# Where VectorE writes the outer product of a step, where ScalarE copies the minus half, and which load goes first: three moves in a fused DFT and two-layer MoE kernel

## The chip, the cores and the metric

The kernel runs on one core of one Trainium2 chip. The metric is the device time of one execution in microseconds (us). Shorter is better. The engines are TensorE (PE), VectorE (DVE), ScalarE (ACT), GpSimd (POOL) and the queue engine SyncE (SP), which issues nearly all DMAs.

## What is computed

```python
X = np.fft.fft(x, axis=1)            # x: 2 x 3008 x 256, fp32
X = np.fft.fft(X, axis=2).real
h = X.reshape(6016, 256) @ w_in1     # 256 -> 2048
y = relu(h)**2 @ w_out1              # 2048 -> 256
h = y @ w_in2
P = a0 + a1*h + a2*h*h + a3*h*h*h
Q = 1 + |b0|*|h| + |b1|*h*h
out = (P / (Q + 1e-6)) @ w_out2
```

## The kernel before, in words

**The transform.** The real part of the 2D DFT is symmetric, so only 3012 columns are worked on: the transform gives two sums per column, and a column and its mirror are `plus + minus` and `plus - minus` in the first layer's hidden values. A matmul in full fp32 is not used: each operand is split into a high part and a low rest (`hi`, `lo`), and each product is three matmuls (lo\*hi, hi\*lo, hi\*hi).

**Tiles and steps.** The columns are 12 tiles of 256 (the last has 196). A tile with its mirror gives 512 tokens. The 2048 hidden values are 16 blocks of 128, taken two at a time, so a tile has 8 units and the kernel has 96 steps (`STEPS`). Step s makes the first layer's unit s, and, ten steps later (`SKEW`), the second layer's unit of the same number. All engines run the same step number side by side from orders that are written out by hand; nothing is scheduled by a planner.

**TensorE in step s** (in this order): `up1(s)`, 12 matmuls of 256 columns, first the minus half (L884), then the plus half (L892); `down1(s-2)`, 12 matmuls of 512 (L868); `up2(s-10)`, 12 matmuls of 512 (L859); `down2(s-12)`, 12 matmuls of 512 (L868). The plus half accumulates onto an outer product that VectorE has written into the same PSUM bank, so it waits for `outer_ready`. `up2` waits until VectorE has read the previous unit's result (`h2_read`), since the second layer's hidden values have one pair of PSUM banks.

**VectorE in step s**: add and subtract of plus and minus (L718, L719), which give the hidden values of 512 tokens; `divide(s-11)`, three instructions (L736, L738: two steps to the reciprocal, L742: the quotient); `outer_product(s+1)`, two instructions (L690); every eighth step `keep_z_lo` (L747), the low part of the first layer's output; `read_h2(s-10)`, three instructions (L725 makes q', L726 and L728 the cubic; L728 is the last reader of the PSUM banks). In steps 0 to 10 `divide` has nothing to do; there the outer product stands directly behind the subtract, and `split1` (L757) makes the low part of the hidden values.

**ScalarE in step s**: ReLU and square (L549, L551), every eighth step `keep_z_hi` (L606), `abs_h2` and `cubic_h2` (L567, L575), which read `up2`'s result, `keep_hi1` (L558), every eighth step `keep_out` (L613), then |q'| (L581), the copy of the next step's minus half out of PSUM (`keep_minus`, L543), and logarithm and exponential (L591, L594), the seed of the reciprocal.

**GpSimd in step s**: the split of the quotient into high and low (L498, L500) as soon as VectorE's L742 is done, then the low part of the first layer's hidden values (L491). Before step 10 it splits the second layer's weights, which come by two DMAs of 2 MB: eight pairs of L463 and L465. TensorE waits for the first four pairs ahead of step 10 and for all eight ahead of step 12.

**SyncE** stores the transform's tiles, and once the last is stored it loads tile 1 back (`load_y(1)`, two DMAs), then the second layer's two weights. The later tiles are loaded from the step loop.

The order of the middle of a step, on VectorE and on ScalarE:

```python
                if before is not None:
                    divide(before)
                if before is not None and unit(s + 1) is not None:
                    outer_product(s + 1)
```

```python
                if second is not None:
                    abs_q(second)
                if unit(s + 1) is not None:
                    keep_minus(s + 1)
                ...
                if second is not None:
                    seed_from_q(second)
```

Of the kernel before, what the change touches and what calls it, by code (L numbers as in the profile page):

```python
# [62 lines left out]
EARLY = TILES - 2  # L63
# [68 lines left out]
def fft_moe_kernel(nc, x, w_in1, w_out1, w_in2, w_out2, coef, f47, fold, twiddle, pair, out_t):  # L132
# [9 lines left out]
    with ctx:  # L142
# [105 lines left out]
        def unit(m):  # L248

            return m if 0 <= m < STEPS else None  # L250

        def pairs(t):

            return min(WIDE, COLUMNS - t * WIDE)
# [67 lines left out]
        def y_of(t):  # L322

            return y_odd if t % Y_BUFS else y_even
# [40 lines left out]
        def after_u_stored(eng, t):  # L365
            eng.wait_ge(u_stored[t % (STAGE_BUFS + 1)], 16 * (t // (STAGE_BUFS + 1) + 1))
# [4 lines left out]
        def _(sp):  # L371
# [3 lines left out]
            def load_w(dst, w, loaded):  # L375
                sp.dma_start(dst[:, :, :], w.rearrange("(k p) f -> p k f", p=P)).then_inc(loaded, 16)
# [13 lines left out]
            def load_y(t):  # L390
                n = pairs(t)
                for v, s in zip(y_d, y_of(t)):
                    sp.dma_start(s[:, :, 0:n].bitcast(F32), v[:, :, t * WIDE:t * WIDE + n]
                                 ).then_inc(y_loaded[t % Y_BUFS], 16)
# [6 lines left out]
            def load_u(t):  # L401
                n = pairs(t)
                after_u_stored(sp, t)
                sp.dma_start(u_s[:, t % Y_BUFS, 0:n], u_d[:, t * WIDE:t * WIDE + n].to_broadcast([P, n])
                             ).then_inc(u_loaded[t % Y_BUFS], 16)

            def store_out(t):
                n = 2 * pairs(t)
                sp.wait_ge(out_kept, t + 1)
                if t < TILES - 1:  # L410
                    sp.dma_start(out_v[:, :, t * TN:t * TN + n], out_s[:, :, 0:n]).then_inc(out_stored, 16)
                    return
                sp.dma_start(out_v[:, 0, t * TN:t * TN + n], out_s[:, 0, 0:n]).then_inc(out_stored, 16)
                sp.wait_ge(upper_kept, 1)
                sp.dma_start(out_v[:, 1, t * TN:t * TN + n], out_s[:, 1, 0:n]).then_inc(out_stored, 16)
# [18 lines left out]
                after_stored(sp, t)  # L434
            for t in range(TILES - STAGE_BUFS - 1, TILES):
                after_u_stored(sp, t)
            load_y(1)
            load_w(w_in2_raw, w_in2, w_in2_loaded)
            load_w(w_out2_raw, w_out2, w_out2_loaded)
            for t in range(1, TILES):  # L440
                sp.wait_ge(plus_ready, t * UNITS)
                if t + 1 < TILES:
                    load_u(t + 1)
                    load_y(t + 1)
                if t >= 3:
                    store_out(t - 3)
# [67 lines left out]
        def _(act):  # L514
# [25 lines left out]
            def keep_minus(m):  # L540
                act.wait_ge(minus_ready, m + 1)
                after(act, diff_done, m)
                nc.scalar.activation(minus_s[:, :, 0:pairs(m // UNITS)], h1_minus(m), ACT.Copy).then_inc(minus_kept, 1)  # L543
# [64 lines left out]
            def keep_out(t):  # L608
                n = 2 * pairs(t)
                after(act, out_stored, 16 * t)  # L610
                if t < TILES - 1:
                    act.wait_ge(prod2_done, (t + 1) * UNITS)
                    nc.scalar.activation(out_s[:, :, 0:n], o_p[:, :, 0:n], ACT.Copy).then_inc(out_kept, 1)  # L613
                else:
                    act.wait_ge(half_done, 1)
                    nc.scalar.activation(out_s[:, 0, 0:n], o_p[:, 0, 0:n], ACT.Copy).then_inc(out_kept, 1)
# [10 lines left out]
            for s in range(STEPS):  # L627
                second, summed, multiplied = unit(s - SKEW), unit(s - LAG1), unit(s - SKEW - LAG2)
                square_relu(s)
                if summed is not None and summed % UNITS == UNITS - 1:  # L630
                    keep_z_hi(summed // UNITS)
                if second is not None:
                    from_h2(second)
                if s >= HEAD:
                    keep_hi1(s)
                if multiplied is not None and multiplied % UNITS == UNITS - 1:
                    keep_out(multiplied // UNITS)
                if second is not None:
                    abs_q(second)
                if unit(s + 1) is not None:  # L640
                    keep_minus(s + 1)
                if s == 0:
                    keep_y_hi(EARLY)
                if second is not None:
                    seed_from_q(second)
                if s < HEAD:
                    keep_hi1(s)
                if s == 0:
                    keep_y_hi(EARLY + 1)
# [19 lines left out]
        def _(dve):  # L669
# [13 lines left out]
            def outer_product(m):  # L683
                t, n = m // UNITS, pairs(m // UNITS)
                if m % UNITS == 0:
                    dve.wait_ge(u_loaded[t % Y_BUFS], 16 * (t // Y_BUFS + 1))
                after(dve, diff_done, m)
                for i in range(2):
                    f = 2 * (m % UNITS) + i
                    nc.vector.tensor_scalar(h1_plus(m)[:, i, :], u_s[:, t % Y_BUFS, 0:n], w_col[:, f:f + 1], None, ALU.mult  # L690
                                            ).then_inc(outer_ready, 1)

            def keep_y_lo(t):
                hi, lo = y_tile(t)
                dve.wait_ge(y_hi_kept, t + 1)
                if t > STAGE_BUFS:
                    after_u_stored(dve, t - STAGE_BUFS - 1)
                nc.vector.tensor_copy(u_stage[:, t % (STAGE_BUFS + 1), 0:pairs(t)], uv_bank(t)[0:1, 1, :]).then_inc(u_kept, 1)
                nc.vector.tensor_tensor(lo, uv_bank(t), hi.bitcast(F32), ALU.subtract).then_inc(y_lo_kept, 1)
# [60 lines left out]
            for s in range(STEPS):  # L760
                second, before, summed = unit(s - SKEW), unit(s - SKEW - 1), unit(s - LAG1)
                add_and_subtract(s)
                if before is None:
                    outer_product(s + 1)
                if s == 1:
                    keep_y_lo(EARLY)
                if 0 < s <= HEAD:
                    split1(s - 1)
                if s == 1:
                    keep_y_lo(EARLY + 1)  # L770
                if before is not None:
                    divide(before)
                if before is not None and unit(s + 1) is not None:
                    outer_product(s + 1)
                if summed is not None and summed % UNITS == UNITS - 1:
                    keep_z_lo(summed // UNITS)
                if second is not None:
                    read_h2(second)
# [219 lines left out]
```

## Time and profile before

| | |
|---|---|
| median of 3 runs | 1044.0 us (1040.78 to 1044.02) |
| the profiled execution's own time | 1043.1 us |
| its span | 1041.3 us |
| TensorE busy, matmul / weight load | 1003.2 us (96%) / 848.1 us |
| VectorE busy | 941.8 us (90%) |
| ScalarE busy | 882.0 us (85%) |
| GpSimd busy | 572.1 us (55%) |
| chain that ended last, by engine | DVE 45%, ACT 28%, issue 15%, PE 9%, POOL 2%, DMA 1% |
| DMA engines, mean share | high in the first 95 us only |

A matmul's end in the profile is modelled and overlaps the next one's start (a 512-column matmul shows 0.39 us and the next starts some 0.23 us behind it), so TensorE's progress is read from the starts. The first step's add starts at 70 us; the steps up to 10 take 4.1 to 4.5 us each, those from 14 on 9.7 us, every eighth of them 10.8 us; behind 954 us the last units of the second layer are drained.

### The profile page before, as it was taken

The numbers are of one execution on the slowest core, as the hardware profiler recorded it, in microseconds if no ns is written. First come the engines' busy times: TensorE is split into PE (matmuls) and PEld (weight loads), VectorE is DVE, ScalarE is ACT, GpSimd is POOL, SyncE is SP. The second block draws the span as 40 slices with busy tenths as digits, with TensorE's granted clock in tenths as the row PEclk, the third lists the DMA queues.
The fourth block names the chain that finished last, engine by engine and source line by source line (L and its number), as shares of the span: only waits on it lengthen the run. The fifth ranks groups of instructions, "written<-read, shape, count | busy, mean of one in ns | idle before, by whom it ended". The sixth has DMA issues, their size and how long they took to land.

```text
span 1041.3 us, 13708 instructions
## 1 busy us (share of the span) xinstructions
PE 1003.2 (96%) x5098; PEld 848.1 (81%) x5098; DVE 941.8 (90%) x1040; ACT 882.0 (85%) x929; POOL 572.1 (55%) x305
## 2 busy tenths in 40 slices
PE   9999889999999999999999999999999999999875
PEld 8798778888888888888888888888888888788775
DVE  2368899999999999999999999999999999999997
ACT  2348879999899999899899999999999999898873
POOL 0143955656556556556556566566565565565342
PEclk9999989999999999999999999999999999999997
DMA  9766000001001001001001001001001000000000
GB/s 247 289 194 236 7 1 27 1 1 47 1 1 46 1 1 46 1 1 46 2 1 46 1 1 46 1 1 46 1 1 40 1 1 21 1 21 1 1 21 15
DMA packets 24174, 38.02 MB, mean 37 GB/s; under 512 B 1694, under 2 KB 18986, under 8 KB 23466
## 3 DMA queue, kind: packets, MB, share of 16 engines
q1 hardware_dynamic: 24060, 37.14, 11.3%
q8 instruction: 40, 0.66, 0.3%
q14 instruction: 26, 0.21, 0.1%
q10 hardware_dynamic: 48, 0.02, 0.0%
HBM read 25.31 MB, written 11.84 MB: 36 GB/s over the span
## 4 chain that ended last, share of the span: by engine, by line
DVE 45%; ACT 28%; issue 15%; PE 9%; POOL 2%; DMA 1%; DVEq 0%; ACTq 0%; SPq 0%
DVE den_s L725 9%; DVE den_s L738 9%; DVE den_s L736 9%; ACT seed_s L594 9%; ACT seed_s L591 8%; DVE g_value L742 8%; ACT minus_s L543 5%; DVE ps L690 4%; PE ps L805 3%; PE ps L825 2%; PE ps L814 1%; ACT g_value L575 1%; PE ps L868 1%; ACT g_value L549 1%; POOL w_in_lo L465 1%
## 5 line engine op out<-in xcount | busy, mean ns | idle before, releaser
L868 PE MATMUL ps<-g_hi,w_out_lo 128*128 128x512 f32 (+1 forms) x764 | 301.6, 395 | 17.3 <-POOL w_in_lo L500 8.0
L868 PE MATMUL ps<-g_hi,w_out_hi 128*128 128x512 f32 (+1 forms) x764 | 300.3, 393 | 0.0
L868 PE MATMUL ps<-g_lo,w_out_hi 128*128 128x512 f32 (+1 forms) x728 | 283.9, 390 | 0.0
L498 POOL CAST g_hi<-g_value 128x1024 fp32r<-128x1024 f32 x86 | 89.6, 1042 | 339.5 <-DVE g_value L742 339.5
L500 POOL TENSOR_TENSOR g_lo<-g_value,g_hi 128x1024 fp32r<-128x1024 f32 x86 | 207.3, 2411 | 6.9
L491 POOL TENSOR_TENSOR g_lo<-g_value,g_hi 128x1024 fp32r<-128x1024 f32 (+1 forms) x86 | 204.6, 2380 | 0.0
L868 PEld LDWEIGHTS ps<-g_hi,w_out_lo 128*128 128x128 f32 x764 | 145.9, 191 | 47.3 <-POOL w_in_lo L500 9.3
L868 PEld LDWEIGHTS ps<-g_hi,w_out_hi 128*128 128x128 f32 x764 | 145.2, 190 | 29.2
L868 PEld LDWEIGHTS ps<-g_lo,w_out_hi 128*128 128x128 f32 x728 | 137.9, 189 | 25.6
L581 ACT ACTIVATE den_s<-den_s 128x1024 f32<-128x1024 f32 x88 | 93.5, 1062 | 62.9 <-DVE den_s L725 62.8
L736 DVE SCALAR_TENSOR_TENSOR den_s<-den_s,seed_s 128x1024 f32<-128x1024 f32 x87 | 107.7, 1238 | 25.3 <-ACT seed_s L594 25.3
L859 PE MATMUL ps<-z_hi,w_in_lo 128*128 128x512 f32 x352 | 110.7, 395 | 8.4 <-DVE g_value L728 8.4
L725 DVE SCALAR_TENSOR_TENSOR den_s<-den_s,b_abs,ps 128x1024 f32<-128x1024 f32 x88 | 112.1, 1273 | 5.3 <-ACT g_value L575 5.0
L742 DVE SCALAR_TENSOR_TENSOR g_value<-g_value,coef_s,den_s 128x1024 f32<-128x1024 f32 x86 | 110.5, 1285 | 3.0
L728 DVE SCALAR_TENSOR_TENSOR g_value<-g_value,coef_s,ps 128x1024 f32<-128x1024 f32 x86 | 110.2, 1281 | 3.0
L738 DVE SCALAR_TENSOR_TENSOR den_s<-den_s,seed_s 128x1024 f32<-128x1024 f32 x87 | 108.6, 1249 | 3.0
L859 PE MATMUL ps<-z_lo,w_in_hi 128*128 128x512 f32 x352 | 109.0, 391 | 0.0
L859 PE MATMUL ps<-z_hi,w_in_hi 128*128 128x512 f32 x352 | 108.6, 390 | 0.0
L549 ACT ACTIVATE g_value<-g_value 128x1024 f32<-128x1024 f32 (+1 forms) x96 | 100.3, 1044 | 7.9 <-DVE g_value L719 7.5
L726 DVE TENSOR_TENSOR g_value<-g_value,ps 128x1024 f32<-128x1024 f32 x86 | 104.5, 1215 | 0.0
L567 ACT ACTIVATE den_s<-ps,coef_s 128x1024 f32<-128x1024 f32 x88 | 97.1, 1103 | 7.8 <-PE ps L859 7.8
L575 ACT ACTIVATE g_value<-ps,coef_s 128x1024 f32<-128x1024 f32 x86 | 103.1, 1199 | 0.0
(118 smaller groups left out, 1894.2 us busy)
## 6 DMA issues: line engine op xcount, KB each, us to landing
x_s<-x SPq DMA_DIRECT2D x16, 384.0 KB, 7.2
out_t<-out_s SPq DMA_DIRECT2D x11, 512.0 KB, 5.7
w_out_unsplit_lo<-w_out SPq DMA_DIRECT2D x2, 2048.0 KB, 18.4
tw_s<-twiddle SPq DMA_DIRECT2D x1, 3012.0 KB, 17.3
y_hi_dram<-y_stage_hi SPq DMA_DIRECT2D x10, 256.0 KB, 3.7
y_lo_dram<-y_stage_lo SPq DMA_DIRECT2D x10, 256.0 KB, 4.5
w_in_raw<-w_in SPq DMA_DIRECT2D x1, 2048.0 KB, 10.5
w_in_unsplit_lo<-w_in SPq DMA_DIRECT2D x1, 2048.0 KB, 9.9
```

The lines of the kernel that those rows point to most:

```text
L491: nc.gpsimd.tensor_tensor(g1_lo_s[:, p, :, 0:n], r_s[:, p, :, 0:n], g1_hi_s[:, m % 2, :, 0:n].bitcast(F32), ALU.subtract).then_inc(pool_lo ...
L500: nc.gpsimd.tensor_tensor(lo, g, hi.bitcast(F32), ALU.subtract).then_inc(g2_lo, 1)
L549: nc.scalar.activation(r, r, ACT.Relu).then_inc(relu_done, 1)
L575: nc.scalar.activation(num_of(m), h2_banks(m)[:, :, 0:width(m)], ACT.Identity, bias=a2, scale=a3).then_inc(cubic_done, 1)
L725: nc.vector.scalar_tensor_tensor(den, den, b_abs[:, 0:1], h2, ALU.add, ALU.mult).then_inc(q_signed, 1)
L726: nc.vector.tensor_tensor(num, num, h2, ALU.mult).then_inc(t_h_done, 1)
L728: nc.vector.scalar_tensor_tensor(num, num, a1, h2, ALU.add, ALU.mult).then_inc(h2_read, 1)
L736: nc.vector.scalar_tensor_tensor(den, den, Q_CONST, seed, ALU.add, ALU.mult).then_inc(t_done, 1)
L738: nc.vector.scalar_tensor_tensor(den, den, 2.0, seed, ALU.subtract, ALU.mult, reverse0=True).then_inc(rec_done, 1)
L742: nc.vector.scalar_tensor_tensor(num, num, a0, den, ALU.add, ALU.mult).then_inc(g2_done, 1)
L859: last = nc.tensor.matmul(h[:, i, 0:n], lhs, rhs, start=(j == 0), stop=(j == len(products) - 1))
L868: last = nc.tensor.matmul(acc[:, mb, 0:n], w[a][:, f, mb * P:(mb + 1) * P], g[c][:, i, 0:n], start=(f == 0 and j == 0), stop=(f == FB - 1 ...
```

## The change

Three moves. On VectorE, `outer_product(s + 1)` stands directly behind the subtract in every step, ahead of `divide`; in step 1 one low part of the transform's (`keep_y_lo`) comes behind `split1` instead of ahead of it. On ScalarE, `keep_minus(s + 1)` comes ahead of `abs_q`. On SyncE, the second layer's weights are loaded ahead of tile 1. No instruction is added, taken away or made larger.

```diff
             for t in range(TILES - STAGE_BUFS - 1, TILES):
                 after_u_stored(sp, t)
-            load_y(1)
             load_w(w_in2_raw, w_in2, w_in2_loaded)
             load_w(w_out2_raw, w_out2, w_out2_loaded)
+            load_y(1)
...
                     keep_out(multiplied // UNITS)
+                if unit(s + 1) is not None:
+                    keep_minus(s + 1)
                 if second is not None:
                     abs_q(second)
-                if unit(s + 1) is not None:
-                    keep_minus(s + 1)
...
                 add_and_subtract(s)
-                if before is None:
+                if unit(s + 1) is not None:
                     outer_product(s + 1)
-                if s == 1:
-                    keep_y_lo(EARLY)
                 if 0 < s <= HEAD:
                     split1(s - 1)
                 if s == 1:
+                    keep_y_lo(EARLY)
                     keep_y_lo(EARLY + 1)
                 if before is not None:
                     divide(before)
-                if before is not None and unit(s + 1) is not None:
-                    outer_product(s + 1)
```

VectorE's instructions from the subtract of step 11 on, before (`g_value` holds first-layer values in L718 and L719 and the second layer's numerator elsewhere; `ps` is PSUM):

```order
L719 TENSOR_TENSOR g_value<-ps,minus_s 128x2x256
L736 SCALAR_TENSOR_TENSOR den_s<-den_s,seed_s 128x1024
L738 SCALAR_TENSOR_TENSOR den_s<-den_s,seed_s 128x1024
L742 SCALAR_TENSOR_TENSOR g_value<-g_value,coef_s,den_s 128x1024
L690 TENSOR_SCALAR ps<-u_s,w_col 128x256 x2
L725 SCALAR_TENSOR_TENSOR den_s<-den_s,b_abs,ps 128x1024
L726 TENSOR_TENSOR g_value<-g_value,ps 128x1024
L728 SCALAR_TENSOR_TENSOR g_value<-g_value,coef_s,ps 128x1024
L718 TENSOR_TENSOR g_value<-ps,minus_s 128x2x256
```

and now, at the same place:

```order
L719 TENSOR_TENSOR g_value<-ps,minus_s 128x2x256
L690 TENSOR_SCALAR ps<-u_s,w_col 128x256 x2
L736 SCALAR_TENSOR_TENSOR den_s<-den_s,seed_s 128x1024
L738 SCALAR_TENSOR_TENSOR den_s<-den_s,seed_s 128x1024
L742 SCALAR_TENSOR_TENSOR g_value<-g_value,coef_s,den_s 128x1024
L725 SCALAR_TENSOR_TENSOR den_s<-den_s,b_abs,ps 128x1024
L726 TENSOR_TENSOR g_value<-g_value,ps 128x1024
L728 SCALAR_TENSOR_TENSOR g_value<-g_value,coef_s,ps 128x1024
L718 TENSOR_TENSOR g_value<-ps,minus_s 128x2x256
```

The pair L690 moved from between the quotient (L742) and L725 to between the subtract (L719) and L736.

ScalarE's instructions of the same step, before:

```order
L558 ACTIVATE g_hi<-g_value 128x1024
L581 ACTIVATE den_s<-den_s 128x1024
L543 ACTIVATE minus_s<-ps 128x512
L591 ACTIVATE seed_s<-den_s,ln_bias 128x1024
L594 ACTIVATE seed_s<-seed_s,exp_bias 128x1024
```

and now:

```order
L558 ACTIVATE g_hi<-g_value 128x1024
L543 ACTIVATE minus_s<-ps 128x512
L581 ACTIVATE den_s<-den_s 128x1024
L591 ACTIVATE seed_s<-den_s,ln_bias 128x1024
L594 ACTIVATE seed_s<-seed_s,exp_bias 128x1024
```

L543 and L581 changed places; nothing else moved on ScalarE.

## Rows read from the trace of the kernel before

**Rows 1.** A plain and a z step: length, PE, PEld, DVE, ACT, POOL busy, PEclk.
```profile
571.08:580.77 9.69, 9.69 (x50) 8.17 (x49) 9.31 (x12) 8.85 (x10) 5.82 (x4) 1.00 0.00 0
580.77:591.59 10.82, 10.38 (x51) 8.34 (x49) 10.44 (x12) 9.75 (x11) 6.97 (x4) 1.00 0.00 0
```
**Rows 2.** Timeline of VectorE, plain step: start, duration, engine, line, operation, [idle before <-releaser].
```profile
571.08 0.69 DVE L718 TENSOR_TENSOR g_value<-ps,minus_s 128x512 f32<-128x512 f32 x1
571.68 0.68 DVE L719 TENSOR_TENSOR g_value<-ps,minus_s 128x512 f32<-128x512 f32 x1
572.63 1.23 DVE L736 SCALAR_TENSOR_TENSOR den_s<-den_s,seed_s 128x1024 f32<-128x1024 f32 x1 [0.27 <-ACT seed_s L594]
...
575.16 1.28 DVE L742 SCALAR_TENSOR_TENSOR g_value<-g_value,coef_s,den_s 128x1024 f32<-128x1024 f32 x1
576.36 0.87 DVE L690 TENSOR_SCALAR ps<-u_s,w_col 128x256 f32<-128x256 f32 x2
577.13 1.27 DVE L725 SCALAR_TENSOR_TENSOR den_s<-den_s,b_abs,ps 128x1024 f32<-128x1024 f32 x1
...
580.77 0.68 DVE L718 TENSOR_TENSOR g_value<-ps,minus_s 128x512 f32<-128x512 f32 x1
```
**Rows 3.** Who waited for whom: total us, times, longest.
```profile
DVE den_s L736 <- ACT seed_s L594: 25.3, 86, 1.1
```
**Rows 4.** Timeline of ScalarE in the same step.
```profile
578.44 1.06 ACT L581 ACTIVATE den_s<-den_s 128x1024 f32<-128x1024 f32 x1 [0.78 <-DVE den_s L725]
579.41 0.58 ACT L543 ACTIVATE minus_s<-ps 128x512 f32<-128x512 f32 x1
```
**Rows 5.** Timeline of TensorE: the first matmul of `up2` behind a z step.
```profile
513.10 0.71 PE L859 MATMUL ps<-z_hi,w_in_lo 128*128 128x512 f32 x2 [0.68 <-DVE g_value L728]
```
**Rows 6.** Timeline of GpSimd, plain step.
```profile
566.81 1.04 POOL L498 CAST g_hi<-g_value 128x1024 fp32r<-128x1024 f32 x1 [3.79 <-DVE g_value L742]
...
570.30 2.41 POOL L491 TENSOR_TENSOR g_lo<-g_value,g_hi 128x1024 fp32r<-128x1024 f32 x1
576.50 1.05 POOL L498 CAST g_hi<-g_value 128x1024 fp32r<-128x1024 f32 x1 [3.79 <-DVE g_value L742]
```
**Rows 7.** Timeline of VectorE, step 11.
```profile
126.41 1.97 DVE L736 SCALAR_TENSOR_TENSOR den_s<-den_s,seed_s 128x1024 f32<-128x1024 f32 x1 [0.27 <-ACT seed_s L594]
128.41 3.25 DVE L738 SCALAR_TENSOR_TENSOR den_s<-den_s,seed_s 128x1024 f32<-128x1024 f32 x1
```
**Rows 8.** Timeline of GpSimd: first and last of the 16 weight splits, first L491.
```profile
93.60 1.04 POOL L463 CAST w_in_hi<-w_in_unsplit_lo 128x1024 fp32r<-128x1024 f32 x1 [29.26 <-DMA w_in_unsplit_lo<-w_in]
...
124.91 2.38 POOL L465 TENSOR_TENSOR w_out_lo<-w_out_unsplit_lo,w_out_hi 128x1024 fp32r<-128x1024 f32 x1
127.25 3.32 POOL L491 TENSOR_TENSOR g_lo<-g_value,g_hi 128x1024 fp32r<-128x1024 f32 x1
```
**Rows 9.** Timeline of TensorE, `up1(12)`: first minus matmul, first plus matmul.
```profile
127.34 0.38 PE L884 MATMUL ps<-y_odd_hi,w_in_lo 128*128 128x256 f32 x1 [1.52 <-POOL w_out_lo L465]
...
133.82 0.58 PE L892 MATMUL ps<-y_odd_hi,w_in_lo 128*128 128x256 f32 x1 [5.50 <-DVE ps L690]
```
**Rows 10.** Busy time by engine just behind that wait (columns as in Rows 1).
```profile
134.00:140.00 6.00, 6.00 (x19) 5.00 (x20) 5.70 (x6) 4.96 (x6) 4.82 (x3) 0.57 0.00 0
```
**Rows 11.** Timeline of the SP queue: the issues that change places.
```profile
82.72 0.36 SPq L393 DMA_DIRECT2D y_odd_hi<-y_hi_dram  x1
...
83.65 0.46 SPq L376 DMA_DIRECT2D w_in_unsplit_lo<-w_in  x1
```
**Rows 12.** DMA issues between 82 and 104 us: KB each, us to landing.
```profile
w_out_unsplit_lo<-w_out SPq DMA_DIRECT2D x1, 2048.0 KB, 14.8
```
**Rows 13.** Timeline of TensorE: `up1(8)`, the first reader of tile 1.
```profile
102.90 0.28 PE L884 MATMUL ps<-y_odd_hi,w_in_lo 128*128 128x256 f32 x1
```
**Rows 14.** Length from step 14's L718 to step 90's, on to 95's; L718 busy.
```profile
158.43:906.22 747.79, 51.73 (x77) 1.00 0.05 15
906.22:953.51 47.29, 2.80 (x6) 1.00 0.03 12
```

## The prediction

> **What bounds the kernel now.** I read the granted clock first (full in both steps below), then the busy times by step, VectorE's timeline, the waits, and the other engines' timelines beside it.
>
> Most of the time is 66 plain steps of 9.69 us and 10 steps of 10.82 us in which the first layer's output is split too (z steps): 66 x 9.69 + 10 x 10.82 = 747.7, and the trace has 747.79 us from step 14's add to step 90's [rows 14]. In a plain step TensorE is busy 9.69 of 9.69 us; in a z step it is not, 10.38 of 10.82 [rows 1]. That missing time stands ahead of `up2`, which waits for VectorE's L728, the last reader of the PSUM banks [rows 5]. So TensorE sets the plain steps, and VectorE the z steps, by 10.82 - 9.69 = 1.13 us each.
>
> VectorE can't catch up in the seven steps between. It stands still for 0.27 us ahead of L736 in every step [rows 2], 86 times, 25.3 us in all, until ScalarE's exponential is done [rows 3]. That wait closes a ring: L725, |q'|, the copy of the minus half, logarithm, exponential, L736, L738, L742, L690, L725. Going round takes one step, 9.69, the same as TensorE's. Two engines are level here, and a third is close: see the port below.
>
> **ScalarE's move.** Ahead of |q'| ScalarE idles 0.78 us for L725, and the minus copy behind it takes 0.58 [rows 4]. Ahead of |q'| the copy fits into the idle time, so the exponential ends some 0.48 earlier (the start-to-start time of L543). Cost nothing, cover 0.78 us.
>
> **VectorE's move.** L690 takes 576.36 to 577.13, 0.78 us [rows 2]. Behind the subtract it fills the 0.27 us hole, and what it has more lies where the exponential no longer waits. I count from the end of L742 (575.16 + 1.28 = 576.44). L725 starts 0.08 before that end, as L690 does now; L725 to the next L718 takes 580.77 - 577.13 = 3.64; L718 and L719 take 571.08 to 572.36, 1.28; L690 0.78 with 0.03 of gap. L736 could start at -0.08 + 3.64 + 1.28 + 0.81 = 5.65. L736 to the end of L742 takes 572.63 to 576.44, 3.81 [rows 2]. VectorE alone would go round in 9.46 us. The exponential is no bound: L725 ends at 1.2, and from |q'| to L736 it is now 578.44 to 582.32 (L736 one step on), 3.88, less 0.48: 4.6, a whole us ahead of 5.65.
>
> **The port between VectorE and GpSimd is what is late next.** GpSimd begins its cast 0.06 behind L742's end (576.50), and its three instructions go from 566.81 to 572.71, 5.90 us [rows 6], so it is done at 5.96. Now L736 comes at 572.63, when it is just over. In the new order it comes at 5.65, on top of L491. What that costs, step 11 shows: there L736, which takes 1.23 elsewhere, took 1.97, and L738 3.25, beside GpSimd [rows 7, 8]. L736 started at 126.41; less its 1.23 it began to work at 127.15, 0.14 before L465's end at 127.29. L738 began to work at 128.41 + 3.25 - 1.23 = 130.43, 0.14 before L491's end at 130.57. So L736 and L738 (two SBUF inputs each) don't share with GpSimd; they wait until 0.14 before its instruction's end. Then L736 works from 5.96 - 0.14 = 5.82, and the round is 5.82 + 3.81 = 9.63 us. Of the 0.27 us hole, only 0.06 is gained in a plain step. Bounds: 9.46 (no block), 9.77 (block to the very end).
>
> The Trainium skill says of this (SBUF — State Buffer, "Who interferes with whom") that a VectorE instruction with two SBUF inputs and a GpSimd instruction that reads SBUF take a shared pair of ports as a lock, and the later one fully blocks until the first has finished. The blocking agrees with step 11. Its "until finished", taken at the instruction's shown end, would make 9.77 of 9.63; step 11 and the present plain step (L736 starts 0.08 before L491's end and takes its usual 1.23) speak for the 0.14.
>
> In a z step L747 puts 1.13 us more on VectorE, not on GpSimd, so the port is long free: 9.46 + 1.13 = 10.59 us.
>
> Steps 14 to 90: 66 x 9.63 + 10 x 10.59 = 741.5, less than 747.8 by **6.3 us**. TensorE could do 76 x 9.69 = 736.4; it no longer sets the pace, it waits some 0.5 us in every z step and never else. Steps 90 to 95 are narrower in the first layer and take 9.46 each [rows 14] with no block (GpSimd's L491 is shorter): 5 x 0.24 = **1.2 us**. Behind step 95 nothing changes.
>
> **The start.** Steps 10 to 13 hang on GpSimd's weight splits. GpSimd waits 29.26 us for the first weights and starts at 93.60; the last split ends at 127.29, and TensorE stands 1.52 us for it [rows 8, 9]. The weights would be issued 0.93 us earlier (82.72 for 83.65 [rows 11]) and go ahead of tile 1's 512 KB. Lower bound 0.9; upper 0.9 plus a quarter of the 9.9 us that `w_in`'s 2048 KB took from issue (83.65) to GpSimd's start, for those 512 KB, 3.4. I take 2.0: the tile's transfer partly ran in the time the weights needed to get going. The splits end at 125.3.
>
> In step 11 TensorE then stood 5.50 us for L690, since it lay behind the three divide instructions that the port held up [rows 9]; behind that wait the granted clock was 0.57 over six us [rows 10], between the full 2.4 GHz and half, 1.2 GHz. Now L690 comes right behind the subtract, at 126.2. L491 runs 125.3 to 127.7, L736 takes the port at 127.5, L742 ends at 131.3, step 12's add starts at 131.3 - 0.08 + 3.64 = 134.9, and step 14's two rounds of 9.63 later, at 154.1. It was 158.43 [rows 14]: **4.3 us** less. With no gain from the weights, L742 ends at 132.98 as now, and by the same working it is 2.6 us.
>
> Tile 1 now comes last. `w_out`, issued right behind `w_in` at 84.1, landed 14.8 later, at 99 [rows 11, 12], with all of these transfers ahead of it; the same bytes in another order end at about the same time, so tile 1 is there at 99 to 100. `up1(8)` reads it at 102.90 [rows 13], perhaps 0.9 us earlier with the swap in step 1 (`split1` first lets TensorE go on earlier). Cost nothing, cover 2 to 4 us. The swap itself ends in front of GpSimd's splits and is worth nothing.
>
> **Sum.** 4.3 + 6.3 + 1.2 = 11.8 us. Against the profiled execution, 1043.1: 1031.3. The median is 0.9 higher: **1032**.
>
> **The rivals.**
> *The port doesn't block so near the end*, or GpSimd gets through earlier: then TensorE sets nearly every step, 736.4 for 741.5, 5 us more gain, 1027. For: VectorE alone needs only 9.46. Against: both long instructions of step 11. Chance 0.12.
> *The start loses its gain to the clock.* TensorE has two idle stretches at about 133 and 142 us (1.5 and 2.9 us, for GpSimd's and VectorE's results) where it had one of 5.5. If the clock falls as it did, six us at 0.57 cost up to 4: 1036. Chance 0.13.
> *The block lasts to the end of L491*: 9.77 in plain steps, 66 x 0.14 = 9.2 less gain: 1041, no change that could be measured. It is the outcome by the page's rule. The rows above speak against it. Chance 0.18.
> *Slower: ScalarE waits for TensorE.* The minus copy now stands ahead of |q'|, and it needs the first half of `up1(s+1)`, which TensorE does last in its step. If that half comes late, |q'|, logarithm and exponential come late, and L736 waits for them again. It decides once the exponential comes later than 5.82, that is with the copy more than 1.1 us behind the end of L725. Were it 1.35 late, plain steps would take 9.88: 66 x 0.25 = 16 us, 1048. Against it: today L543 shows no wait, and TensorE has no idle time ahead of that half in plain steps. Chance 0.08.
>
> The forecast has 0.49.
>
> **How the numbers follow.** 0.3% (3.1 us, about what a measurement of this kernel can tell from no change) puts the border at 1040.9. Faster: the forecast, the first two rivals, and a quarter of the third, 0.79. Same: the rest of the third, 0.13. Slower: 0.08. The range takes in the forecast with its bounds, 1027 less 2, and the third rival up to the border: 1025 to 1041.
>
> **What would show it.** L736's duration: above 1.23, near 1.4, in plain steps with no wait on the exponential. L742's end to L742's end: 9.63 in plain steps, 10.59 in z steps. ScalarE's idle time for L725 gone or far below 0.78. TensorE's first `up2` matmul idle 0.3 to 0.6 in z steps. GpSimd's first split at about 91.6. L690 of step 11 at 126 and no wait of 5.5 us on it. Step 14's add at 154. A plain step that is still 9.69 with L736 undisturbed would mean that TensorE sets it and the port reading was wrong; a wait ahead of L543 would mean the slower rival.

## The result and the profile after

The changed kernel takes **1032.3 us** (median of 4 runs, 1031.93 to 1032.47) where the kernel before takes 1043.4 beside it (1040.78 to 1044.02): the ratio is 0.9898, with a 95% interval of 0.988 to 0.9916. The forecast was 1032, range 1025 to 1041. The profiled execution has a span of 1030.7 us for 1041.3. Three single executions in the runs below took far longer than the others of their kernel (2.0 ms for the kernel before, 1107.63 us with the loads' order alone, 5.6 ms with both halves on ScalarE); they are in the medians but not in the ratios.

The page of the changed kernel, busy time by engine:

```profile
PE 1001.2 (97%) x5098; PEld 847.3 (82%) x5098; DVE 954.1 (93%) x1040; ACT 901.1 (87%) x929; POOL 571.7 (55%) x305
```

VectorE shows 12 us more busy time than before, with the same instructions. Those are not work. Most of them are L736, 116.5 us in 87 instructions for 107.7, as the next rows show; L757 has 2.8 more in the first ten steps, and L738 2.0 less. The lines behind L690 keep their numbers below line 760; TensorE's are three lower than before (L856 is `up2`, L865 `down`, L881 and L889 the two halves of `up1`).

**The plain step**, VectorE's timeline, answering to [rows 2]:

```profile
564.74 0.68 DVE L718 TENSOR_TENSOR g_value<-ps,minus_s 128x512 f32<-128x512 f32 x1
565.34 0.68 DVE L719 TENSOR_TENSOR g_value<-ps,minus_s 128x512 f32<-128x512 f32 x1
566.05 0.88 DVE L690 TENSOR_SCALAR ps<-u_s,w_col 128x256 f32<-128x256 f32 x2
566.84 1.41 DVE L736 SCALAR_TENSOR_TENSOR den_s<-den_s,seed_s 128x1024 f32<-128x1024 f32 x1
568.28 1.22 DVE L738 SCALAR_TENSOR_TENSOR den_s<-den_s,seed_s 128x1024 f32<-128x1024 f32 x1
569.54 1.28 DVE L742 SCALAR_TENSOR_TENSOR g_value<-g_value,coef_s,den_s 128x1024 f32<-128x1024 f32 x1
570.74 1.28 DVE L725 SCALAR_TENSOR_TENSOR den_s<-den_s,b_abs,ps 128x1024 f32<-128x1024 f32 x1
...
574.38 0.68 DVE L718 TENSOR_TENSOR g_value<-ps,minus_s 128x512 f32<-128x512 f32 x1
```

and GpSimd's beside it, answering to [rows 6]:

```profile
564.74 2.42 POOL L491 TENSOR_TENSOR g_lo<-g_value,g_hi 128x1024 fp32r<-128x1024 f32 x1
570.89 1.04 POOL L498 CAST g_hi<-g_value 128x1024 fp32r<-128x1024 f32 x1 [3.73 <-DVE g_value L742]
```

There is no idle time ahead of L736 any more, and no wait for the exponential (of 86 such waits 2 are left, 1.4 us together, both behind step 95's add); instead L736 takes 1.41 us for 1.23. Its median is 1.35. It starts at 566.84 while L491 runs until 567.16. Less its own 1.22 it began to work at 567.03, 0.13 us before L491's end. Between steps 12 and 90 there are 59 L736 that are longer than 1.25 us, and by the same working all began 0.12 to 0.15 us before L491's end. The step is 574.38 - 564.74 = 9.64 us.

**The z step** from TensorE's side, the first matmul of `up2` in the two steps behind one, answering to [rows 5]:

```profile
194.56 0.70 PE L856 MATMUL ps<-z_hi,w_in_lo 128*128 128x512 f32 x2 [0.25 <-DVE g_value L728]
...
204.36 0.62 PE L856 MATMUL ps<-z_hi,w_in_lo 128*128 128x512 f32 x2
```

The wait is 0.25 us for 0.68. From `up2` to `up2`, that tile has six distances of 9.69 us, one of 10.11 and one of 9.80 (194.56 to 204.36), together 78.05 us for about 78.65.

**The start.** VectorE's step 11 [rows 7], GpSimd's splits and first L491 [rows 8], TensorE's `up1(12)` [rows 9]:

```profile
126.05 0.88 DVE L690 TENSOR_SCALAR ps<-u_s,w_col 128x256 f32<-128x256 f32 x2
126.83 1.22 DVE L736 SCALAR_TENSOR_TENSOR den_s<-den_s,seed_s 128x1024 f32<-128x1024 f32 x1
128.08 1.23 DVE L738 SCALAR_TENSOR_TENSOR den_s<-den_s,seed_s 128x1024 f32<-128x1024 f32 x1
```

```profile
90.41 1.04 POOL L463 CAST w_in_hi<-w_in_unsplit_lo 128x1024 fp32r<-128x1024 f32 x1 [26.59 <-DMA w_in_unsplit_lo<-w_in]
...
124.29 2.42 POOL L491 TENSOR_TENSOR g_lo<-g_value,g_hi 128x1024 fp32r<-128x1024 f32 x1
```

```profile
126.98 0.39 PE L889 MATMUL ps<-y_odd_hi,w_in_lo 128*128 128x256 f32 x1 [0.56 <-DVE ps L690]
...
143.94 0.74 PE L856 MATMUL ps<-z_hi,w_in_lo 128*128 128x512 f32 x2 [2.35 <-DVE g_value L728]
144.53 0.92 PE L856 MATMUL ps<-z_lo,w_in_hi 128*128 128x512 f32 x2
145.24 1.06 PE L856 MATMUL ps<-z_hi,w_in_hi 128*128 128x512 f32 x2
```

TensorE's wait of 5.50 us for L690 is 0.56. GpSimd starts 3.2 us earlier, so L491 is past before L736 comes, and neither L736 nor L738 is held up. Further on TensorE stands 2.35 us at 143.94, and then two matmuls take 0.59, 0.71 and 0.85 us, start to start, where they take 0.46 at full clock. The granted clock is 1.00 from 141 to 143.9, and 0.50, the half clock, from 145 to 148.

By stages, between the starts of VectorE's L718 in the profiled executions (us). "Vector", "scalar" and "weights" are the three moves alone, described below:

| stretch | before | after | vector | scalar | weights | vector + scalar |
|---|---|---|---|---|---|---|
| start to step 10 | 114.4 | 114.2 | 114.2 | 114.9 | 114.0 | 114.4 |
| steps 10 to 14 | 44.06 | 40.41 | 42.07 | 44.94 | 40.79 | 42.89 |
| steps 14 to 90 | 747.79 | 742.98 | 742.69 | 745.22 | 747.75 | 742.86 |
| steps 90 to 95 | 47.29 | 45.85 | 45.89 | 46.65 | 47.28 | 45.91 |
| step 95 to the end | 87.8 | 87.3 | 87.2 | 87.7 | 85.7 | 86.9 |

The first and last rows have the same work in the same order (but for the swap in step 1 and the order of the loads) in all six and still differ by up to 2 us, so single profiled executions are compared by the rows between. The row of steps 10 to 14 holds the clock as well: step 13 took 10.77 us in the changed kernel and 10.62 with vector + scalar, behind a fall of the clock, and 9.58 with vector alone, where the clock stayed full.

### The profile page after: what moved, and what is told of

Read it like the earlier page. It is cut to its first block, busy times and chain, and to the rows that moved or that the text cites. A ratio compares the mean times of both kernels' runs of the same rounds, so it can differ in the third digit from the quotient of the medians.

```text
span 1030.7 us, 13708 instructions
## 1 busy us (share of the span) xinstructions
PE 1001.2 (97%) x5098; PEld 847.3 (82%) x5098; DVE 954.1 (93%) x1040; ACT 901.1 (87%) x929; POOL 571.7 (55%) x305
## 4 chain that ended last, share of the span: by engine, by line
DVE 47%; PE 41%; issue 10%; ACT 2%; DVEq 0%; ACTq 0%
PE ps L865 20%; PE ps L856 10%; DVE den_s L736 7%; DVE den_s L725 7%; DVE den_s L738 6%; DVE g_value L726 6%; DVE g_value L742 6%; DVE g_value L718 4%; DVE g_value L719 3%; DVE ps L690 3%; PE ps L802 3%; PE ps L889 3%; PE ps L881 3%; PE ps L822 2%; PE ps L811 1%
## 5 line engine op out<-in xcount | busy, mean ns | idle before, releaser
L865 PE MATMUL ps<-g_hi,w_out_lo 128*128 128x512 f32 (+1 forms) x764 | 300.9, 394 | 16.9 <-POOL w_in_lo L500 9.5
L865 PE MATMUL ps<-g_hi,w_out_hi 128*128 128x512 f32 (+1 forms) x764 | 299.8, 392 | 0.0
L865 PE MATMUL ps<-g_lo,w_out_hi 128*128 128x512 f32 (+1 forms) x728 | 283.2, 389 | 0.0
L498 POOL CAST g_hi<-g_value 128x1024 fp32r<-128x1024 f32 x86 | 89.5, 1041 | 333.2 <-DVE g_value L742 333.2
L500 POOL TENSOR_TENSOR g_lo<-g_value,g_hi 128x1024 fp32r<-128x1024 f32 x86 | 207.9, 2418 | 6.9
L491 POOL TENSOR_TENSOR g_lo<-g_value,g_hi 128x1024 fp32r<-128x1024 f32 (+1 forms) x86 | 203.5, 2367 | 0.0
L865 PEld LDWEIGHTS ps<-g_hi,w_out_lo 128*128 128x128 f32 x764 | 145.5, 190 | 47.4 <-POOL w_in_lo L500 10.8
L865 PEld LDWEIGHTS ps<-g_hi,w_out_hi 128*128 128x128 f32 x764 | 145.0, 190 | 29.2
L865 PEld LDWEIGHTS ps<-g_lo,w_out_hi 128*128 128x128 f32 x728 | 137.4, 189 | 25.5
L725 DVE SCALAR_TENSOR_TENSOR den_s<-den_s,b_abs,ps 128x1024 f32<-128x1024 f32 x88 | 112.4, 1277 | 6.7 <-ACT g_value L575 4.9
L736 DVE SCALAR_TENSOR_TENSOR den_s<-den_s,seed_s 128x1024 f32<-128x1024 f32 x87 | 116.5, 1339 | 1.4 <-ACT seed_s L594 1.4
L856 PE MATMUL ps<-z_hi,w_in_lo 128*128 128x512 f32 x352 | 110.9, 396 | 6.6 <-DVE g_value L728 6.6
L549 ACT ACTIVATE g_value<-g_value 128x1024 f32<-128x1024 f32 (+1 forms) x96 | 100.1, 1043 | 16.6 <-DVE g_value L719 14.8
L742 DVE SCALAR_TENSOR_TENSOR g_value<-g_value,coef_s,den_s 128x1024 f32<-128x1024 f32 x86 | 110.5, 1285 | 3.0
L856 PE MATMUL ps<-z_lo,w_in_hi 128*128 128x512 f32 x352 | 109.5, 393 | 0.0
L738 DVE SCALAR_TENSOR_TENSOR den_s<-den_s,seed_s 128x1024 f32<-128x1024 f32 x87 | 106.6, 1225 | 3.0
L856 PE MATMUL ps<-z_hi,w_in_hi 128*128 128x512 f32 x352 | 109.1, 391 | 0.0
L575 ACT ACTIVATE g_value<-ps,coef_s 128x1024 f32<-128x1024 f32 x86 | 103.2, 1200 | 0.0
L551 ACT ACTIVATE g_value<-g_value 128x1024 f32<-128x1024 f32 (+1 forms) x96 | 100.4, 1046 | 3.0
## 6 DMA issues: line engine op xcount, KB each, us to landing
w_in_raw<-w_in SPq DMA_DIRECT2D x1, 2048.0 KB, 10.7
```

Of the source, the lines that this page charges most:

```text
L491: nc.gpsimd.tensor_tensor(g1_lo_s[:, p, :, 0:n], r_s[:, p, :, 0:n], g1_hi_s[:, m % 2, :, 0:n].bitcast(F32), ALU.subtract).then_inc(pool_lo ...
L500: nc.gpsimd.tensor_tensor(lo, g, hi.bitcast(F32), ALU.subtract).then_inc(g2_lo, 1)
L551: nc.scalar.activation(r, r, ACT.Square).then_inc(g1_done, 1)
L575: nc.scalar.activation(num_of(m), h2_banks(m)[:, :, 0:width(m)], ACT.Identity, bias=a2, scale=a3).then_inc(cubic_done, 1)
L725: nc.vector.scalar_tensor_tensor(den, den, b_abs[:, 0:1], h2, ALU.add, ALU.mult).then_inc(q_signed, 1)
L736: nc.vector.scalar_tensor_tensor(den, den, Q_CONST, seed, ALU.add, ALU.mult).then_inc(t_done, 1)
```

## The experiments

All times are medians beside the kernel before on the same chip; the ratio to it follows with its interval.

### The three moves apart

**VectorE's move alone:**

```diff
                 add_and_subtract(s)
-                if before is None:
+                if unit(s + 1) is not None:
                     outer_product(s + 1)
...
                     divide(before)
-                if before is not None and unit(s + 1) is not None:
-                    outer_product(s + 1)
```

(with the swap in step 1).

> Only VectorE's move. Theory A (the idle time ahead of L736 is gone as soon as L690 lies in it; the exponential, even with the minus copy still behind |q'|, is ready 5.1 us behind L742's end, ahead of the port's 5.8): the step loop is as with the whole change, plain steps 9.63 to 9.70 us and the step behind a z step 9.45, some 5 us less from step 14 to 90; the 5.5 us wait of step 11 is gone, but the weight splits end at 127.3 as before, so the start gives 2 to 3 us. Sum: 1035 to 1036. Theory B (the exponential still ends the wait, and ScalarE's move is what frees VectorE): L736 waits again, the steps stay at 9.69 and 10.8, and only the start's 2 to 3 us come: 1041.

Measured: 1033.9 us, 0.9925 (0.9908 to 0.9943). Theory A in its mechanism, and 1 us below its range (steps 90 to 95 give 1.4 us that its sum leaves out). Steps 14 to 90 take 742.7 us, as with the whole change. ScalarE's move adds nothing to it.

**ScalarE's move alone:**

```diff
-                if second is not None:
-                    abs_q(second)
                 if unit(s + 1) is not None:
                     keep_minus(s + 1)
+                if second is not None:
+                    abs_q(second)
```

> Only ScalarE's move. Theory A (the ring through the exponential is cut from this side as well; VectorE then comes 5.65 us behind L742's end to the same port): L736 stretches to about 1.4 us, z steps and the step behind them together 20.2 us instead of 20.5, 4 to 5 us less from step 14 to 90, nothing at the start, since L690 still stands behind the divide instructions in step 11: 1037 to 1039. Theory B (the hole has to be filled by L690 to be worth anything): no change, 1043.

Measured: 1038.8 us, 0.9966 (0.9952 to 0.9981). Theory A in its mechanism. The VectorE timeline of this kernel, in a plain step and with L690 at its old place:

```profile
288.12 0.68 DVE L719 TENSOR_TENSOR g_value<-ps,minus_s 128x512 f32<-128x512 f32 x1
288.86 1.35 DVE L736 SCALAR_TENSOR_TENSOR den_s<-den_s,seed_s 128x1024 f32<-128x1024 f32 x1
```

L736 comes right behind the subtract and is held up by the port here as well. The waits of this kernel still have the exponential, though, 24 times for 86:

```profile
DVE den_s L736 <- ACT seed_s L594: 10.2, 24, 1.1
```

One step in eight is 10.1 us long, that behind the step in which ScalarE also copies the output out of PSUM (`keep_out`): there L736 waits 0.68 us for the exponential. With L690 ahead of L736 that step takes 9.64, so the copy is covered; without, it costs 0.4 us a tile. So the gain from step 14 to 90 is 2.6 us, not 4.8. (The profiled execution, 1041.19 us, is the slowest of the twelve, which go from 1037.1 up.)

**The order of the loads alone:**

```diff
-            load_y(1)
             load_w(w_in2_raw, w_in2, w_in2_loaded)
             load_w(w_out2_raw, w_out2, w_out2_loaded)
+            load_y(1)
```

> Only the loads' order. GpSimd's splits start 2 to 3 us earlier and end near 124.5. L491 of step 10 is then past before L738 needs the port, so TensorE's wait for L690 in step 11 shrinks from 5.5 us by about 2.5. The step loop is unchanged. Theory A (the start is worth what GpSimd's end moves): 1040 to 1041. Theory B (the start hangs on VectorE's order, the weights alone only move a wait): 1042 to 1043.5.

Measured: 1038.2 us, 0.9961 (0.9947 to 0.9976). That is more than either theory gave. Steps 10 to 14 take 3.3 us less. TensorE still waits 4.76 us for L690 in step 11, where about 3 were expected, but the port is nearly free:

```profile
126.14 1.47 DVE L736 SCALAR_TENSOR_TENSOR den_s<-den_s,seed_s 128x1024 f32<-128x1024 f32 x1 [0.27 <-ACT seed_s L594]
127.64 1.23 DVE L738 SCALAR_TENSOR_TENSOR den_s<-den_s,seed_s 128x1024 f32<-128x1024 f32 x1
```

L736 and L738 take 1.47 and 1.23 us for the 1.97 and 3.25 of [rows 7]. The earlier splits let L491 end at 126.53, just behind L736's start at 126.14, and so out of the divide instructions. The clock has a part too: it is back at 1.00 by 135, where before the change it was 0.50 until 139, and step 12 takes 10.57 us for 11.43. The step loop is unchanged at 747.75 us.

**VectorE's and ScalarE's moves, without the loads:**

> Everything but the loads' order. The weights' share is what this lacks against the whole change (1032.3). Theory A (splits end at 127.3, L736 takes the port ahead of L491 and L738 is held up behind it, step 12's add comes at 136.5 instead of 134.2): 1034 to 1035, equal to VectorE's move alone. Theory B (GpSimd's splits aren't on the path once TensorE has its outer product): 1032.5.

Measured: 1033.8 us, 0.9924 (0.9907 to 0.9941). Theory A: the same as VectorE's move alone. Against the whole change (1032.3), the loads are worth 1.5 us here by the medians and 2.7 by the ratios, whose intervals overlap; steps 10 to 14 have 2.5 of it. Alone they were worth some 4. Both moves shorten the same stretch of step 11, so their gains don't add up.

### The port, shorter and longer

**GpSimd's L491 as a cast** in the whole change, 1.04 us for 2.42:

```diff
-                nc.gpsimd.tensor_tensor(g1_lo_s[:, p, :, 0:n], r_s[:, p, :, 0:n],
-                                        g1_hi_s[:, m % 2, :, 0:n].bitcast(F32), ALU.subtract).then_inc(pool_lo1, 1)
+                nc.gpsimd.tensor_copy(g1_lo_s[:, p, :, 0:n], r_s[:, p, :, 0:n]).then_inc(pool_lo1, 1)
```

> The whole change, with GpSimd's L491 as a plain cast (1.04 us for 2.41; the low part of the hidden values is the value itself, not the rest, so the output is another). GpSimd is off the port 1.4 us sooner, ahead of L736. Theory A (the port and TensorE are nearly level, and TensorE's 9.69 us is what sets the steps): L736 is back at 1.22 us, VectorE catches up in two or three steps instead of five, the tile is still 77.9 to 78.1 us long, the time 1031 to 1032.5. Theory B (the port sets the step loop): plain steps fall below 9.64 on all engines, a tile to 77.5 or less, the time to 1027 or less.

Measured: 1030.2 us, 0.9898 (0.9883 to 0.9914), a ratio equal to that of the whole change. Its VectorE and GpSimd timelines:

```profile
566.35 1.22 DVE L735 SCALAR_TENSOR_TENSOR den_s<-den_s,seed_s 128x1024 f32<-128x1024 f32 x1
...
568.86 1.28 DVE L741 SCALAR_TENSOR_TENSOR g_value<-g_value,coef_s,den_s 128x1024 f32<-128x1024 f32 x1
570.30 1.28 DVE L724 SCALAR_TENSOR_TENSOR den_s<-den_s,b_abs,ps 128x1024 f32<-128x1024 f32 x1
```

```profile
564.07 1.04 POOL L491 CAST g_lo<-g_value 128x1024 fp32r<-128x1024 f32 x1
```

Theory A: L735 (L736 in the others) is back at 1.22, and what VectorE gains there it loses 2.5 us later, standing 0.16 us ahead of L724 (570.14 to 570.30), which comes 0.12 us behind the end of ScalarE's L574; ScalarE in turn waited 0.18 us for TensorE in that step. The tile takes 78.05 us as before. Taking the block away from L736 is worth nothing, since TensorE's 9.69 us is right behind it.

**More work on the port**, three copies of 32 x 128 between L500 and L491:

```diff
+                for _ in range(3):
+                    more[0] += 1
+                    pool.wait_ge(more_done, more[0] - 1)
+                    nc.gpsimd.tensor_copy(w_rows[:, :], w_rows[:, :]).then_inc(more_done, 1)
                 nc.gpsimd.tensor_tensor(g1_lo_s[:, p, :, 0:n], r_s[:, p, :, 0:n],
```

> The whole change, with three short extra GpSimd copies (32 x 128) between L500 and L491 in every step from 10 on, together x us. Theory A (the round L742, GpSimd's three instructions, L736 is closed by the port): L736 stretches by x, and a plain step gets 9.64 + x us; z steps, where GpSimd is done 1.1 us before L736, change only by what x is over that. Theory B (the stretch of L736 is not a wait for GpSimd's end): L736 keeps 1.35 and the steps 9.65 to 9.70.

Measured: 1100.2 us, 1.0567 (1.0552 to 1.0583). GpSimd's and VectorE's timelines (L744 is L736 here):

```profile
567.93 0.98 POOL L498 COPY w_rows<-w_rows 32x128 f32<-32x128 f32 x3
568.88 2.40 POOL L499 TENSOR_TENSOR g_lo<-g_value,g_hi 128x1024 fp32r<-128x1024 f32 x1
```

```profile
569.26 0.88 DVE L698 TENSOR_SCALAR ps<-u_s,w_col 128x256 f32<-128x256 f32 x2
570.05 2.31 DVE L744 SCALAR_TENSOR_TENSOR den_s<-den_s,seed_s 128x1024 f32<-128x1024 f32 x1
```

The three copies put off L499 by 0.95 us, L744 takes 2.31 for 1.36 to 1.41, and plain steps take 10.55 us for 9.64: 0.91 more. L744 less its own 1.22 began to work at 571.14; L499 ended at 571.28. That is 0.14 us before the end, as in step 11 before the change. Theory A, with the size: on the far side of the balance, 0.95 us of GpSimd time costs 0.91 us a step. A z step takes 11.7 us for 10.7, and the one behind it 9.45 in both kernels.

### What ends a z step

The stand of TensorE in z steps, 0.42 us from `up2` to `up2` and 0.11 in the next, is what is left. I tried to take it away.

**Half of the outer product of the z step on ScalarE:**

```diff
+            def outer_half(m):
+                t, n, f = m // UNITS, pairs(m // UNITS), 2 * (m % UNITS) + 1
+                act.wait_ge(u_loaded[t % Y_BUFS], 16 * (t // Y_BUFS + 1))
+                act.wait_ge(outer_ready, 2 * m + 1)
+                nc.scalar.activation(h1_plus(m)[:, 1, :], u_s[:, t % Y_BUFS, 0:n], ACT.Copy, scale=w_col[:, f:f + 1]
+                                     ).then_inc(outer_ready, 1)
...
+                if unit(s + 1) is not None and on_scalar(s + 1):
+                    outer_half(s + 1)
                 if unit(s + 1) is not None:
                     keep_minus(s + 1)
...
-                for i in range(2):
+                for i in range(1 if on_scalar(m) else 2):
```

> The whole change, with the second half of the outer product of a z step (one in eight, ten in all) on ScalarE, behind its L558. VectorE has 0.39 us less in each z step. Theory A (z steps are VectorE's, and TensorE stands 0.4 to 0.5 us in each): that stand nearly goes, 0.3 to 0.4 us in each of ten z steps, 1028.5 to 1029.5. Theory B (ScalarE, which has its own extra copy in that step, becomes late): the exponential or L575 ends the wait in its place, no gain, 1032 to 1034.

Measured: 1039.6 us, 0.9983 (0.9972 to 0.9994), by the ratios 0.9% worse than without. Neither theory named what happened. VectorE, ScalarE and TensorE in one z step (their L703, L749, L553 and L902 are L690, L736, the new half, and `up1`'s plus half):

```profile
263.54 0.49 DVE L703 TENSOR_SCALAR ps<-u_s,w_col 128x256 f32<-128x256 f32 x1
263.93 1.61 DVE L749 SCALAR_TENSOR_TENSOR den_s<-den_s,seed_s 128x1024 f32<-128x1024 f32 x1
```

```profile
269.95 0.48 ACT L553 ACTIVATE ps<-u_s,w_col 128x256 f32<-128x256 f32 x1
```

```profile
270.49 0.39 PE L902 MATMUL ps<-y_odd_hi,w_in_lo 128*128 128x256 f32 x1 [1.15 <-ACT ps L553]
```

VectorE gave up 0.39 us and got it back as a longer wait for the port, since in the z step itself L736 still meets L491; only the L736 of the step behind doesn't. And ScalarE wrote its half 1.15 us after TensorE wanted it. The z step itself is still 10.7 us; the loss lies in the step behind, 10.13 us for 9.45, where VectorE's L738 (L725 elsewhere) waits 0.58 us for ScalarE, and it comes in every tile: together some 5.4 of the 6.7 us by which steps 14 to 90 are longer (749.6 for 743.0). **Both halves on ScalarE** (the same edit with `range(0 if on_scalar(m) else 2)` on VectorE and both halves behind a wait for the subtract):

> As the run before, with both halves on ScalarE. VectorE has 0.78 us less in a z step, more than TensorE's stand. Theory A: TensorE's stand ahead of up2 is gone, every step is TensorE's, 1027.5 to 1029, no more than 1 us better than one half. Theory B (ScalarE is full): L725 waits for L575 or L736 for the exponential, worse than one half, 1030 to 1034.

Measured: 1045.5 us, 1.0041 (1.0025 to 1.0056), worse again, and outside both theories. The profiled execution is the one of 5.6 ms; TensorE is busy through all of it at a granted clock of 1.00, the reason is unknown, and the place of the loss can't be read from it.

**Half of L747**, VectorE's extra work in a z step:

```diff
+                k = n // 2 if 0 < t < TILES - 1 else n
-                nc.vector.tensor_tensor(z_tile(t)[1][:, :, 0:n], z_banks(t)[:, :, 0:n],
-                                        z_tile(t)[0][:, :, 0:n].bitcast(F32), ALU.subtract).then_inc(z_lo, 1)
+                nc.vector.tensor_tensor(z_tile(t)[1][:, :, 0:k], z_banks(t)[:, :, 0:k],
+                                        z_tile(t)[0][:, :, 0:k].bitcast(F32), ALU.subtract).then_inc(z_lo, 1)
```

> The whole change, with VectorE's L747 on half of its columns in tiles 1 to 10 (the low part of the other half is left stale, so the output is another): 0.53 us less on VectorE in each z step. Theory A (a z step is VectorE's alone, as the prediction had it): TensorE's stand ahead of up2, 0.4 to 0.5 us, goes, z steps 10.2 us, the time 1028 to 1028.5. Theory B (ScalarE's high part L606, which waits for TensorE's last up2 matmul, holds L567, L575 and so L725 at the same level): L725 then waits for L575, z steps stay at 10.6 to 10.7, the time 1031.5 to 1032.5.

Measured: 1031.7 us, 0.9889 (0.9866 to 0.9912), no difference from the whole change. Theory B. VectorE and ScalarE in that kernel's z step (L748 is L747):

```profile
189.73 0.69 DVE L748 TENSOR_TENSOR z_lo<-ps,z_hi 128x512 fp32r<-128x512 f32 x1
190.49 1.28 DVE L725 SCALAR_TENSOR_TENSOR den_s<-den_s,b_abs,ps 128x1024 f32<-128x1024 f32 x1
```

```profile
187.25 1.03 ACT L606 ACTIVATE z_hi<-ps 128x1024 fp32r<-128x1024 f32 x1
188.18 1.11 ACT L567 ACTIVATE den_s<-ps,coef_s 128x1024 f32<-128x1024 f32 x1
189.17 1.21 ACT L575 ACTIVATE g_value<-ps,coef_s 128x1024 f32<-128x1024 f32 x1
```

L748 is half a us shorter, but L725 starts 0.11 us behind the end of L575 (190.38) all the same. In the changed kernel it starts 0.12 us behind it in the same step.

**Half of L606, ScalarE's extra work, with L747 whole:**

```diff
+                k = n // 2 if 0 < t < TILES - 1 else n
-                nc.scalar.activation(z_tile(t)[0][:, :, 0:n], z_banks(t)[:, :, 0:n], ACT.Copy).then_inc(z_hi, 1)
+                nc.scalar.activation(z_tile(t)[0][:, :, 0:k], z_banks(t)[:, :, 0:k], ACT.Copy).then_inc(z_hi, 1)
```

> The whole change, with only ScalarE's L606 on half of its columns in tiles 1 to 10 (the other half of the high part is left stale, so the output is another), VectorE's L747 whole. Theory A (ScalarE alone holds the z step, and VectorE has room): the same gain as with both halves, z steps 10.24 us, 1027 to 1028. Theory B (the two are level): L747 holds L725 where L575 held it, z steps 10.6 to 10.7 us, 1031 to 1032.5.

Measured: 1032.5 us, 0.9911 (0.9891 to 0.9931). Theory B: no gain either. ScalarE's L575 now ends 0.47 us ahead of L725 in that step, and L725 follows straight on L747. **Both halves together:**

> As the run before, with ScalarE's L606 on half of the columns as well, some 0.4 us less on ScalarE in each z step. Theory A: nothing more than the run before. Theory B (VectorE and ScalarE are level in a z step and only both together move it): the stand shrinks from 0.42 us to nearly nothing, z steps 10.2 us, the time 1028 to 1028.5.

Measured: 1027.1 us, 0.9848 (0.9829 to 0.9867). Steps 14 to 90 take 738.3 us, a z step 10.24. TensorE at the same place as above (L858 is `up2`), with no wait left:

```profile
194.16 0.40 PE L867 MATMUL ps<-g_hi,w_out_hi 128*128 128x512 f32 x1
194.39 0.70 PE L858 MATMUL ps<-z_hi,w_in_lo 128*128 128x512 f32 x2
```

Theory B: after the change a z step is held by VectorE and ScalarE at the same level, and 5 us come only when both are relieved.

## Why the prediction was right, and where not

**The wait and what takes its place: right.** Of the 86 waits of L736 for the exponential 2 are left; L736 stretches to 1.41 us ("near 1.4"; 1.35 in the median), and VectorE's plain step is 9.64 (9.63 forecast). The moment at which the port is let go, 0.14 us before GpSimd's end, was read from step 11 and came back as 0.13 and 0.14 in two kernels. The Trainium skill's rule (SBUF — State Buffer, "Who interferes with whom") is right that the later instruction fully blocks: 0.95 us more of GpSimd made 0.91 us more of step. Read as a block to the very end it would have given 9.77 us and 1041; the trace decided by 0.14 us a step.

**A z step: right in size.** Forecast were 9.63 + 10.59 = 20.2 us for a z step and the one behind it, and it is 10.7 + 9.45 = 20.1. The place was off by one step: in the z step itself L736 still meets L491 (1.28 us), and it is the step behind, which starts 1.1 us late for VectorE alone, that has the port free. And the step "TensorE sets the plain steps, and VectorE the z steps" was only half the truth for the new kernel: ScalarE holds them too, which the runs with halves showed. It didn't change the sum. It does change what to do next.

**TensorE "no longer sets the pace": wrong in words.** All its plain distances are 9.69 us. VectorE, at 9.64, only catches up what it lost in the z step. A tile is 78.05 us counted on either engine, because TensorE's wait absorbs the difference.

**Steps 14 to 90: 4.8 us for 6.3, over-sized.** A usual tile is 78.05 for the 78.0 of the forecast, which over 9.5 tiles is half a us. The rest is in single steps of 9.8 to 10.0, and one z step of 11.0, where the usual ones are 9.45 to 9.65 and 10.7. They are nine steps apart (41, 50, 59, 68, 77, 86), and in five of them the profile has 0.20 to 0.30 us ahead of VectorE's L725 in which it waited for nothing that is shown. Before the change the same steps from 50 on are longer too, but only by 0.04 to 0.06 us, except for step 77 with 0.3. So something small was there before and costs more now. That the idle time on VectorE and ScalarE had absorbed it is likely, but what it is was not tried.

**The start: 3.9 us for 4.3** (step 14's add at 154.58 for 158.43; the forecast was 154.1), by two errors that nearly cancel. The term of the loads was under-sized: GpSimd starts 3.2 us earlier, near the upper bound of 3.4, not 2.0. On the other side TensorE's idle time near 142 came as the second rival said, 2.35 us, and the clock fell to half behind it: step 13 took 10.77 us for 9.63. That rival happened, and cost 1.2 us: in the run with half of L747, where the clock stayed full, step 13 took 9.59. It had been priced at up to 4, though six us at 0.57 are only 2.6 us of clock.

**The loads' share** was put at 1.7 us beside the other moves and measured at 1.5 to 2.7. **Steps 90 to 95** gave 1.4 for 1.2. **Tile 1** landed at 98.2, in time for 102.4, as forecast. **ScalarE's move** was costed at nothing and is worth nothing once L690 lies ahead of L736; that it would bring half of the loop's gain by itself was not in the prediction. **The slower rival** (ScalarE behind TensorE) showed as 53 waits of L543, 14.4 us together, 0.4 at most, and never reached L736 in the step loop.

**The sum: partly luck.** From one profiled execution to the other the change gave 10.6 us (1043.1 to 1032.5), where 11.8 were forecast. The forecast then added 0.9 us to come from the profiled execution to the median. The changed kernel's median, 1032.3, doesn't lie above its profiled execution, so that 0.9 was not there, and it hid most of the 1.2 us by which the terms were over-sized.

## What to carry to other kernels

Before filling an engine's idle time, ask which second thing ends it: here the exponential and GpSimd's hold on the port ended within 0.1 us of each other, and only 0.05 us of a 0.27 us hole was to be had. Where three or four rings are level, a step gets shorter only by what they all allow, and the gain shows in the steps that carry extra work. Two moves that shorten the same stretch from two sides are to be measured apart and together; their gains don't add up.

## What the runs showed of the hardware that was not expected

The issue of a DMA can itself be held up. In the changed kernel the SP queue issued tile 1's first load behind 4 MB of weights, and the issue took 7.84 us where it takes 0.36 [rows 11]:

```profile
83.44 0.46 SPq L376 DMA_DIRECT2D w_out_unsplit_lo<-w_out  x1
83.95 7.84 SPq L393 DMA_DIRECT2D y_odd_hi<-y_hi_dram  x1
91.84 0.62 SPq L393 DMA_DIRECT2D y_odd_lo<-y_lo_dram  x1
```

Nothing was waiting in that queue until 99.6, so it cost nothing here; a short load behind it would have been late by those 7.8 us.

The same idle stretches of TensorE were followed by a fall of the clock in one run and by none in another. In the changed kernel the granted clock went to 0.50 behind a stretch of 2.35 us, with two of 0.56 and 0.91 us in the 17 us before. In the run with half of L747 TensorE stood 0.57, 0.89 and then 2.33 us:

```profile
145.36 0.73 PE L857 MATMUL ps<-z_hi,w_in_lo 128*128 128x512 f32 x2 [2.33 <-DVE g_value L728]
145.92 0.63 PE L857 MATMUL ps<-z_lo,w_in_hi 128*128 128x512 f32 x2
```

The granted clock stayed at 1.00 there, and step 13 took 9.59 us for 10.77. VectorE's move alone and VectorE's and ScalarE's together are such a pair too: a last stretch of 2.33 us in both, with step 13 at 9.58 us and full clock in one, and at 10.62 us with the clock down to 0.59 from 146 to 149 in the other. With the loads alone the clock stayed full until behind a stretch of 4.76 us; before the change it was at 0.50 already within one of 5.50, where one of 1.52 had just gone by. What decides between the two outcomes is not shown by these runs. It is worth about 1 us here.
